# Weight splits in an idle stretch of VectorE, its counts beside the gathers, and the rows of single-tile experts ahead of weights

## What is computed

```python
# 1: attention, B=2, H=8, S=768, D=64; keys kept: the first 4 (sinks) and a window of 128
scores = (q @ k.T) / sqrt(D);  a = softmax(where(keep, scores, -1e9));  x = a @ v   # (1536, 512)
# 2: dense expert layer, d_ff = 2048
h = x @ w_in;  g = maximum(h, 0) + alpha * minimum(h, 0);  y = g @ w_out            # (1536, 512)
# 3: top-1 routing over 8 experts, capacity 384, hidden 1024
logits = y @ w_gate;  e = argmax(logits);  gate = softmax(logits)[e]
out[i] = gate[i] * (maximum(y[i] @ w1[e[i]], 0) @ w2[e[i]])   # if its place in e is under capacity
```

## Time and profile before

| | us |
|---|---|
| median of 3 runs | 593.57 (591.67 to 594.1) |
| profiled execution | 591.26 |
| its span | 589.5 |
| busy in it: TensorE | 573.1 |
| weight loads | 495.0 |
| VectorE | 357.5 |
| ScalarE | 269.4 |
| GpSimd | 168.0 |

### The profile page before, as it was taken

The page is one execution under the profiler, slowest core; times in us unless marked ns, Lnnn a source line. Parts: engine busy times, 40 slices in busy tenths (PEclk is TensorE's granted clock), DMA queues, the critical chain, the costliest instruction groups (busy, mean ns, idle before and its releaser), DMA issues.

```text
span 589.5 us, 11767 instructions
## 1 busy us (share of the span) xinstructions
PE 573.1 (97%) x3988; PEld 495.0 (84%) x3988; DVE 357.5 (61%) x1051; ACT 269.4 (46%) x672; POOL 168.0 (29%) x260
## 2 busy tenths in 40 slices
PE   8999999999999999999999999998999999999994
PEld 7788888888888888888888899986989889889882
DVE  5878886575556565765657445456639469398410
ACT  5876654342343335333433121124539477597421
POOL 6435772222121222223123200005202245334110
PEclk9999999999999999999999999999999999999998
DMA  7536452001053302010000060005868769699000
GB/s 197 142 79 189 131 146 72 2 19 39 19 161 90 90 19 72 20 37 19 38 0 19 2 215 1 0 38 155 285 205 286 272 180 395 215 334 347 29 24 17
DMA packets 73357, 67.78 MB, mean 115 GB/s; under 512 B 42900, under 2 KB 49060, under 8 KB 73280
## 3 DMA queue, kind: packets, MB, share of 16 engines
q1 hardware_dynamic: 68464, 57.50, 30.8%
q0 software_dynamic: 3760, 9.03, 5.1%
q10 hardware_dynamic: 1056, 0.26, 0.2%
HBM read 58.01 MB, written 12.06 MB: 119 GB/s over the span
## 4 chain that ended last, share of the span: by engine, by line
PE 91%; DVE 3%; ACT 2%; issue 2%; POOL 0%; POOLq 0%; ACTq 0%; DVEq 0%
PE bank L1123 23%; PE bank L1125 23%; PE bank L1124 23%; PE bank L1113 11%; PE bank L1198 4%; PE bank L1167 4%; PE bank L1271 2%; DVE rw L1578 1%; PE bank L1213 1%; ACT rw L823 0%; PE bank L1297 0%; DVE fw L1797 0%; DVE fw L1802 0%; ACT fw L910 0%; DVE rw L1874 0%
## 5 line engine op out<-in xcount | busy, mean ns | idle before, releaser
L1123 PE MATMUL bank<-rw,wh 128*128 128x256 f32 x512 | 149.1, 291 | 1.2 <-ACT rw L1010 1.2
L1123 PE MATMUL bank<-wh,rw 128*128 128x512 f32 (+1 forms) x368 | 144.4, 392 | 0.6 <-DVE rw L1741 0.2
L1125 PE MATMUL bank<-rw,wl 128*128 128x256 f32 x512 | 144.6, 282 | 0.0
L1124 PE MATMUL bank<-rw,wh 128*128 128x256 f32 x512 | 144.2, 282 | 0.0
L1125 PE MATMUL bank<-wh,rw 128*128 128x512 f32 (+1 forms) x368 | 140.8, 383 | 0.0
L1124 PE MATMUL bank<-wl,rw 128*128 128x512 f32 (+1 forms) x368 | 140.7, 382 | 0.0
L956 ACT CAST rw<-fw 128x256 fp32r<-128x256 f32 x95 | 38.6, 406 | 143.5 <-DVE fw L1802 140.3
L1123 PEld LDWEIGHTS bank<-rw,wh 128*128 128x128 f32 x512 | 97.0, 189 | 4.3 <-issue 1.4
L1124 PEld LDWEIGHTS bank<-rw,wh 128*128 128x128 f32 x512 | 97.0, 189 | 1.7
L1125 PEld LDWEIGHTS bank<-rw,wl 128*128 128x128 f32 x512 | 96.8, 189 | 0.0
L1557 DVE TENSOR_TENSOR wl<-fw,wh 128x512 fp32r<-128x512 f32 x113 | 74.4, 699 | 15.1 <-ACT wh L811 14.9
(11 more groups left out here) (153 smaller groups left out, 677.9 us busy)
## 6 DMA issues: line engine op xcount, KB each, us to landing
fw<-in_moe_w_dram SPq DMA_DIRECT2D x95, 256.0 KB
v_raw<-in_moe_w_dram SPq DMA_DIRECT2D x22, 256.0 KB
fw<-in_moe_w_in_dram SPq DMA_DIRECT2D x16, 256.0 KB, 3.3
fw<-in_moe_w_out_dram SPq DMA_DIRECT2D x16, 256.0 KB, 3.0
y_scratch<-fw SPq DMA_DIRECT2D x12, 256.0 KB, 2.0
out_dram<-v_or_route SPq DMA_DIRECT2D x12, 256.0 KB, 3.6
v_raw<-in_v_dram SPq DMA_DIRECT2D x11, 256.0 KB, 3.6
o_sb<-in_q_dram SPq DMA_DIRECT2D x11, 256.0 KB, 3.3
```

The costliest lines, as they stand in the source:

```text
L1123: pe.matmul(dst, ah, bh, start=start, stop=False, skip_group_check=True)
L1124: pe.matmul(dst, ah, bl, start=False, stop=False, skip_group_check=True)
L1125: return pe.matmul(dst, al, bh, start=False, stop=stop, skip_group_check=True)
```

## The change

In the opening of the experts:

- VectorE splits piece 0 ahead of the copy of y, 1 and 2 where 0 and 1 were (FIRST = 3). Its value loads come right after the ids, then `first_x_low(0)`, piece 3, `first_x_low(1)`, and pieces 4 to 11.
- ScalarE splits pieces 2 and 3 ahead of `router_exp`, and 4 to 7 after it.
- SyncE loads pieces 11, 12 and 13 before its waits, and piece 10 after gather 1 instead of ahead of that wait.
- GpSimd's gather of row 0 waits for the first half of the last y tile's products (`last_first_y_done`) instead of the last router's first step, and names only the first 128 rows of the scratch tensor as its source.
- TensorE makes 6 and 7 placeholders around `slot_T(1)`, not 10 and 10.

In each expert after the first, where it is a single tile: ScalarE splits only pieces 0 and 1 of the next expert ahead of the previous output's scaling and the next rows (it was 0 to 3), and 2 and 3 between its two quarters of ReLU. VectorE splits 0 and 1 ahead of the next rows, and 2 to 9 after `hidden_low`. For pairs the order is as it was.

```diff
--- before.py
+++ after.py
@@ -295,7 +295,7 @@
         CHOSEN, RANKED, PLACED = 7, 10, 24
         LAST_CHOSEN, LAST_PLACED = 6, 22
         NIX = 4
-        FIRST = 2
+        FIRST = 3
 
         NP1 = 2 * PPH
         FP1, FP2 = F1 // PIECE, F2 // PIECE
@@ -599,8 +599,8 @@
                 if p == NP1 + STG2 + FIRST:
                     sp.wait_ge(output_zeroed, 16 * NT)
                     sp.wait_ge(index_steps, NIX)
+                    sp.wait_ge(tokens_gathered[1], 16)
                     load_piece(NP1 + STG2 - 1)
-                    sp.wait_ge(tokens_gathered[1], 16)
                 load_piece(p)
 
 
@@ -726,11 +726,11 @@
             pool.wait_ge(scores_masked, NH)
             pool.wait_ge(y_stored, 16 * TPC * (NC - 1))
             pool.wait_ge(first_row_made, 1)
-            pool.wait_ge(router_steps, RS * (NC - 1) + 1)
+            pool.wait_ge(last_first_y_done, 1)
             pool.indirect_dma_start(
-                out=x_slot[GR - 1], out_offset=None, in_=y_dram,
+                out=x_slot[GR - 1], out_offset=None, in_=y_dram[0:P, :],
                 in_offset=bass.IndirectOffsetOnAxis(ap=first_row[:, 0:1], axis=0),
-                bounds_check=N - 1, oob_is_err=False).then_inc(rows_read_ahead, 16)
+                bounds_check=P - 1, oob_is_err=False).then_inc(rows_read_ahead, 16)
             pool.wait_ge(y_stored, 16 * NT)
             pool.wait_ge(index_steps, 1)
 
@@ -974,6 +974,7 @@
 
             each_step(step)
             evac_yT(NT - TPC)
+            some(2, KC, 0)
             router_exp(NC - 1)
 
             def x_high(i, skipped=0):
@@ -1029,7 +1030,7 @@
                                scale=inv[:, 1, i:i + 1]).then_inc(expert_out_scaled, 1 + skipped)
 
             W1, W2 = KC * FP2, PPH
-            some(FIRST, W1, 0)
+            some(KC, W1, 0)
             busy = Busy(act)
             busy.load(range(E))
             first_x_high(0)
@@ -1056,7 +1057,7 @@
                         some(0, W1 - 2, e + 1)
                     with act.Else():
                         relu(first, 0)
-                        some(0, 4, e + 1)
+                        some(0, 2, e + 1)
                     busy.last_of(e - 1, scaled)
                 with busy.over(e, 1):
                     if e:
@@ -1100,6 +1101,8 @@
                     if e == 0:
                         some(W1 + 4, W2, 0)
                     relu_quarter(first, 0)
+                    if e:
+                        some(2, 4, e + 1)
                     relu_quarter(first, 1)
                     some(4 if e else 0, W1 + 2, e + 1)
                     single_last_high(e)
@@ -1514,13 +1517,13 @@
 
             pe.wait_ge(index_steps, 2)
             slot_T(0)
-            keep_busy(10, H_BANK[0])
+            keep_busy(6, H_BANK[0])
             for e in range(E):
                 first = TPE * e
                 with busy.over(e, 1):
                     if e == 0:
                         slot_T(1)
-                        keep_busy(10, H_BANK[0])
+                        keep_busy(7, H_BANK[0])
                     pair_in(e, 0)
                 with pe.Else():
                     expert_in(first, 0)
@@ -1825,15 +1828,16 @@
                         weights_low(NP1 + e * PPH + p)
 
             each_step(head_step)
+            some(0, 1, 0)
             dve.wait_ge(y_stored, 16 * TPC * (NC - 1))
             dve.wait_ge(y_transposed, TPC * (NC - 1))
             dve.wait_ge(y_done, NF * NC)
             dve.tensor_copy(y_sb[:, TPC - 1, :], Y_BANK[TPC - 1][:, :]).then_inc(last_y_evacuated, 1)
-            some(0, 1, 0)
+            some(1, 2, 0)
             dve.wait_ge(logits_done, NC - 1)
             dve.wait_ge(y_transposed, NT)
             dve.tensor_copy(yT[:, TPC - 1, :, :], yT_bank(NT - 1)[:, :].rearrange("p (c n) -> p c n", c=KC)).then_inc(last_yT_evacuated, 1)
-            some(1, FIRST, 0)
+            some(2, FIRST, 0)
             choose(NC - 1)
             rank(NC - 1)
             dve.wait_ge(experts_counted, 1)
@@ -1880,10 +1884,10 @@
                                          op0=ALU.max, op1=ALU.subtract).then_inc(expert_hidden_low_split, 1)
 
             W1, W2 = KC * FP2, PPH
-            some(FIRST, W1, 0)
             busy = Busy(dve)
             busy.load(range(E // 2))
             first_x_low(0)
+            some(FIRST, KC, 0)
 
             def next_tile(e, skipped):
                 if e + 1 < E:
@@ -1899,13 +1903,13 @@
                 if e == 0:
                     with busy.over(0, 1):
                         first_x_low(1)
-                    some(W1, W1 + 4, 0)
+                    some(KC, W1 + 4, 0)
                     busy.load(range(E // 2, E))
                 else:
-                    some(0, 4, e + 1)
+                    some(0, 2, e + 1)
                 with busy.over(e, 1):
                     if e:
-                        some(4, W1, e + 1)
+                        some(2, W1, e + 1)
                     for b in range(4):
                         pair_low(e, b)
                         if e == 0:
@@ -1935,7 +1939,7 @@
                     hidden_low(first, 0, 2)
                     if e == 0:
                         some(W1 + 4, W2, 0)
-                    some(4 if e else 0, W1 + 2, e + 1)
+                    some(2 if e else 0, W1 + 2, e + 1)
                     single_last_low(e)
                     some(W1 + 2, W2, e + 1)
 
```

## The result

| | before | after |
|---|---|---|
| median, first series (16 runs each) | 592.38 us (591.12 to 595.82) | 596.24 us (594.41 to 599.5) |
| profiled execution | 591.26 us | 594.58 us |
| its span | 589.5 us | 592.9 us |

The ratio is 1.0058, 95% interval 1.0040 to 1.0076: 0.6% or 3.4 us slower (3.4 us by the spans too, 3.9 by the medians), where 1.1 faster was forecast. The same program, timed twice more, gave 0.9973 (0.9948 to 0.9998) and 0.9992 (0.9970 to 1.0014). The first series doesn't agree with these two within the intervals, and most of what follows is about telling the change from what one series of it had besides.

The account below looks back on a forecast made before the run. TensorE, busy for 97% of the span, was taken to bound the kernel. Opening -0.5, expert 5 -1.1, given back +0.5 sum to -1.1 us: 592.5 against the median 593.57, with a range of 590.4 to 594.7.

Parts of the forecast that it names:

- The range: Whole kernel: the forecast's own 592.0 to 593.0, widened to 590.4 to 594.7 since three runs before lay 2.4 us apart.
- The opening, -0.5: Opening of the experts: earlier gathers and fewer placeholders bring the first product to about 411.05, -0.5 us, bounds -0.2 and -0.6.
- the 0.2 from the router chain: Opening: row 0's gather ends before the router begins, so counts and TensorE's value loads come 0.2 us earlier.
- The stop of 0.4 behind the seven placeholders: Opening: seven placeholders end near 410.7, so TensorE stands still for 0.4 before the first product.
- nothing waited: Experts 2 and 4: no waits before; pieces 2 and 3 now just in time, bounds 0 and +0.4, taken as 0.
- Expert 5, -1.1: Single-tile expert 5: next rows no longer stand behind piece 2's load, -1.1 us, bounds 0 and -1.39.
- What is given back, +0.5: Expert 6: DMA-paced pieces hold the last pair_low while TensorE comes earlier, +0.5 us, bounds 0 and +0.85.
- Rival 3, the ring: Stages freed later in experts 2, 4 and 5 delay expert 6's pieces: TensorE 0.75 us later, 594.3; chance 0.17.
- The clock: Granted clock under 1 after 408; the only case said to reach a change of 3 us; chance 0.03.

Follow-up runs that it names:

- r1: The changed kernel, unchanged, executed once more for a second trace: 591.03 us.
- r2: The changed kernel, unchanged, executed once more for a third trace: 590.51 us.
- r5: The changed kernel timed again in five rounds (second series): 591.27 us against 592.32 for the kernel before, ratio 0.9973.
- r6: The changed kernel timed a third time in five rounds, loaded anew (third series): 592.25 us against 593.22 for the kernel before, ratio 0.9992.
- e4: The kernel before without the seven placeholders ahead of the last chunk's table products: 594.88 us, ratio 1.0026.
- r3: The kernel before, unchanged, executed once more for a second trace: 594.07 us.
- e2: The kernel before with 6 and 7 placeholders around slot_T(1) instead of 10 and 10, nothing else: 593.0 us, ratio 0.9988.

## Why the prediction was wrong

**The sign and size of the first series.** No step had them. What fails against it is the assumption under all of the opening, that ScalarE's cast follows `slot_T(1)` by the 0.42 of the rows of before, so that it comes at 409.9 and the first product at 411.05. Here the cast took 3.14 and came at 412.93, the product at 413.82, and in expert 5 `single_last_high` followed its transposes by 3.71. Against the first trace of the kernel before the table gives +2.40 to the end of expert 3, -1.11 from there to expert 6 (the forecast gain), +1.97 to its output and 0.00 behind it: 3.26 of the 3.4. Against the later traces of the change the two holds cost 5.15 - 2.59 = 2.56 us in the opening and 19.62 - 17.48 = 2.14 in expert 6's column. The prediction named no such rival. The repeats show that it would have been one of the execution more than of the change: in two further series and two single executions of the same program it never came. That it was absent in all 13 later runs doesn't prove that the change has no part in its chance; it does show that the change is not enough. **What held the signals stays open.** The range failed for the same reason: it took the spread of three runs for the spread between series.

**The opening, -0.5.** Its steps held in the later traces: L1687, both gathers, `slot_T(1)` 1.1 us behind `slot_T(0)`, first product 2.57 to 2.60 after it. Against 2.97 that is 0.4; the 0.2 from the router chain cannot be told from shifts of the same size ahead of it (`slot_T(0)` lies at 408.55 to 409.46 in the changed traces). Gather 1 was forecast 1.0 earlier and was 0.6 earlier in the first series, which still hid it. The stop of 0.4 behind the seven placeholders was 0.1 at most. What failed is the sum: the gain was carried through expert 3, where "nothing waited". The list of waits doesn't show a margin. In expert 3 the last `pair_low` ended at 498.06 + 0.68 = 498.74, and TensorE wanted it at the seventh block, 495.17 + 18 x 0.23 = 499.31: 0.6 of margin, of which the table leaves 0.4 (10.14 against 9.71 to 9.76). The change takes more than that: TensorE came 0.85 earlier in the second series and VectorE 0.36 later. The other two traces of the kernel before had no margin at all there. I worked out that margin for expert 6 and not for expert 3, which has the same order of work. So the 0.5 was worth nothing at the end of expert 3.

**Expert 5, -1.1.** Right in its mechanism. TensorE's wait for L1010 is gone in all traces of the change, and in the four later ones one of 0.3 to 0.5, once 1.0, stands in its place, mostly for a subtraction of L1557 (now L1560); the stretch from the quarters of expert 5 (from 522.84 in the first trace) to expert 6's first products fell from 4.33 and 4.28 to 3.4 to 3.6, once 4.1: -0.7 in the mean, where -1.1 was forecast. One trace of before has a wait of 2.66 there behind piece 3, and from the end of expert 3 to column 4 it takes 2.5 and 3.1 us more than the other two; no trace with the edit waits more than 1.02. The edit takes the rows out from behind piece 3, so it should be worth more when that piece is late; that it is, is argued, since no run has the same late piece with and without it. Where piece 1 is late, as in the kernel before with 6 and 7, the rows stand behind it in both orders.

**What is given back, +0.5.** Right in place and cause (`pair_low` of expert 6, pieces at the DMA's pace), with a size of 0, 0.3, 1.1 and 1.6, mean 0.7, against bounds of 0 and 0.85. The margin was mis-sized, 0.4 and not 0.75 (the last column against the end of `pair_low`), and the bound let the pieces stay where they were: in the second series the last `pair_low` ended 0.8 later than in the first trace of before, and with TensorE 1.2 earlier that makes 1.2 - 0.4 + 0.8 = 1.6.

**Rival 3, the ring,** was named for expert 6 and priced at +0.75. Pieces did come later in expert 6 in one series, but the runs don't speak for the ring as the cause: the change without the single-tile edits, which frees the stages as before, has its expert 6 as slow (27.1). The DMA share in 513 to 515 doesn't tell either: it was 0.08 in the first trace of before and 0.23 in that of the change, but 0.33 in the third trace of before and 0.34 in the opening alone.

**The clock,** the last of the rivals with 0.03, is out for the change: TensorE was busy for 1.34 us of 4 in 410 to 414 of the first series, the granted clock of that stretch and of the next ones is 1.00, and no later trace of the change has a fall there. No run shows that fewer placeholders around `slot_T(1)` lower the clock: the kernel before with 6 and 7 has 1.00 in 403 to 414 too. Falls are real all the same. In the kernel before and its variants the clock fell to 0.50 at the stops of 2.66 and 2.67 us ahead of expert 6, and in the opening without the seven placeholders, behind a stop of 1.98. What brings them on is not shown: in the first series a stop of 2.66 us passed at 1.00.

**What the change is worth.** By the table: 0 from the opening, -0.8 to expert 6's first products, +0.7 in expert 6 (means of four against two), so about -0.1 us where no piece of expert 6 is late, and -3.1 against the trace where one was, 1.6 of which is the clock. The second and third series have medians 1.05 and 0.97 us under the kernel before, near the -1.1 of the forecast. That nearness is luck: the terms were wrong one by one, and one series of three is at +3.9. The clock goes with these medians. Of the 52 runs of the kernel before in the two series 17 have a mean granted clock of 0.990 or less, and their medians (594.7 and 594.3) lie 2.5 and 2.1 us over those of the others (592.1 and 592.3); of the 24 runs of the change 3 have. Among the others the change is 0.9 and 0.1 faster. Whether the edits make such falls rarer is not shown: 3 of 24 against 17 of 52 is few, and a run's mean doesn't say where the clock fell.

## What to carry to other kernels

A gain at one place must be followed through every later stage that a stream of loads paces, and for each of them the margin has to be worked out (when the last dependent piece ends against when it is wanted), in more than one trace; a list of waits shows only where the margin is already gone. Work that is due should not stand behind work that waits for a load: here one profile showed a stop of 1.2 us at that place and another 2.7, with the clock at 0.50 for 3 us behind it. The mean clock of every run should be read before medians are compared. And a change of 0.2% should be timed in more than one series, since those of one program differed by 0.8% here, more than the intervals within a series.

## What the runs showed of the hardware

- First series (`after`): TensorE's transposes start at 409.79, ScalarE's cast of their result at 412.93, 3.14 behind them, with 3.17 idle ahead of it that the timeline puts down to "remote". In the four later traces of the program (`r1`, `r2`, `r5`, `r6`) the cast is 0.42 behind. In expert 5 it is 535.17 against 531.46, 3.71, and 0.63 or 0.64 in the four.
- Queue "q8 instruction": 44 packets of 16 KB in `after`, 21 of them between 404 and 590, in the kernel before as well. Counted from `slot_T(0)` and without the time of the holds they lie within some 2 us of the same places in `after` and `r6`.
- The load that waits for gather 1 went out 2.3 to 2.5 us after the end of that gather's issue in five traces and 4.4 in one (`e4`), and loads of weights took 7.39 and 9.2 us from issue to landing in the chain of the second series (DMA share 1.01 in 521 to 545).
- A stop of 2.66 us left the granted clock at 1.00 once (first series, at 411); stops of 2.66 and 2.67 us that end at 528.56 and 528.51 had it at 0.50 for about 3 us in two other traces (`r3`, `e2`), from 530.0 and from 528.1, which cost 1.6 and 1.3 us.
- A gather's issue on GpSimd took 1.30 and 1.50 us beside VectorE's six subtractions of pieces from 404.02 on, 1.00 behind them, and 1.42 beside four such subtractions in `r1` (at 412.22); L1687 of VectorE took 0.17 us and under such an issue 0.42.
